# Linear attention and two gated MLPs on one core: one loop over all chunks, the narrow tile fourth in layer one, moved copies

## The reference

```python
q_s = softmax(q, axis=-1); k_s = softmax(k, axis=2)        # exp(. - max) / (sum + 1e-9)
kv = einsum('bhsd,bhse->bhde', k_s, v)
x = einsum('bhsd,bhde->bhse', q_s, kv)  -> [B * S, H * D]
h = x @ w_in;  r = max(h, 0);  x = (s * r * r + b) @ w_out                       # layer one
h = x @ w_in2; sp = log1p(exp(min(h, 20))); out = (h * tanh(sp)) @ w_out2        # layer two
```

## Time and profile before

| | us |
|---|---|
| median of 3 runs | 891.26 (889.41 to 893.04) |
| profiled execution | 890.38 |
| its span, first to last instruction | 888.6 |
| TensorE busy | 865.1 (97%) |
| VectorE busy | 613.5 (69%) |
| ScalarE busy | 378.7 (43%) |
| GpSimd busy | 26.6 (3%) |
| mean granted TensorE clock | 0.988 of full |

### The profile page before, as it was taken

How to read it: one execution, slowest core, us unless ns; L and a number is a source line. 1 busy time by engine, 2 the same in 40 slices (tenths; PEclk the granted TensorE clock), 3 DMA queues, 4 the chain that set the end, 5 groups by cost and what they waited for, 6 DMA issues and landing times.

```text
span 888.6 us, 11126 instructions
## 1 busy us (share of the span) xinstructions
PE 865.1 (97%) x4132; PEld 717.5 (81%) x4132; DVE 613.5 (69%) x1037; ACT 378.7 (43%) x621; POOL 26.6 (3%) x30
## 2 busy tenths in 40 slices
PE   9789999999999999999999899998999999999998
PEld 4578888888888888888997678897888788878886
DVE  8787776665475554222466889688797779778975
ACT  4445433332333323222356555455454445445443
POOL 2300000000000000000000000000000000000000
PEclk9799999999999999999999999999999999999999
DMA  9921111111111100000153000100000000000001
GB/s 227 339 53 40 25 29 28 41 41 41 41 40 40 40 0 1 1 1 0 49 190 143 1 0 1 48 1 1 25 1 0 12 36 0 0 28 19 0 0 48
DMA packets 60645, 36.15 MB, mean 41 GB/s; under 512 B 48320, under 2 KB 50368, under 8 KB 60608
## 3 DMA queue, kind: packets, MB, share of 16 engines
q1 hardware_dynamic: 60608, 35.66, 14.2%
HBM read 30.93 MB, written 4.72 MB: 40 GB/s over the span
## 4 chain that ended last, share of the span: by engine, by line
PE 80%; DVE 11%; ACT 6%; issue 2%; POOL 1%; DMA 0%; DVEq 0%; ACTq 0%
PE H L796 38%; PE Y L810 21%; PE Y L824 17%; PE H L763 2%; PE H L784 2%; ACT t L458 1%; DVE g L702 1%; DVE t L674 1%; ACT t L460 1%; DVE wout_lo L598 1%; DVE t L679 1%; ACT wout_hi L360 1%; DVE t L684 1%; PE H L775 1%; DVE win_lo L598 1%
## 5 line engine op out<-in xcount | busy, mean ns | idle before, releaser
L796 PE MATMUL H<-xs_hi,win_hi 128*128 128x512 f32 (+1 forms) x640 | 240.8, 376 | 7.7 <-DVE g_raw L697 3.3
L796 PE MATMUL H<-xs_hi,win_lo 128*128 128x512 f32 (+1 forms) x640 | 236.8, 370 | 0.0
L796 PE MATMUL H<-xs_lo,win_hi 128*128 128x512 f32 (+1 forms) x640 | 236.7, 370 | 0.0
L824 PE MATMUL Y<-wout_hi,g 128*128 128x512 f32 x576 | 190.1, 393 | 5.4 <-DVE g L702 5.4
L810 PE MATMUL Y<-g,wout_hi 128*128 128x512 f32 (+1 forms) x640 | 183.3, 371 | 0.7 <-DVE g L582 0.7
L796 PEld LDWEIGHTS H<-xs_hi,win_hi 128*128 128x128 f32 x640 | 121.4, 190 | 30.0 <-DVE g_raw L697 4.0
L796 PEld LDWEIGHTS H<-xs_hi,win_lo 128*128 128x128 f32 x640 | 121.3, 190 | 20.8
L796 PEld LDWEIGHTS H<-xs_lo,win_hi 128*128 128x128 f32 x640 | 121.4, 190 | 20.4
L824 PEld LDWEIGHTS Y<-wout_hi,g 128*128 128x128 f32 x576 | 108.7, 189 | 30.9 <-DVE g L702 8.7
L810 PEld LDWEIGHTS Y<-g,wout_hi 128*128 128x128 f32 x640 | 115.2, 189 | 20.1 <-DVE g L582 0.9
L577 DVE SCALAR_TENSOR_TENSOR g_raw<-g_raw,s_col 128x512 f32<-128x512 f32 (+1 forms) x80 | 55.5, 694 | 96.4 <-ACT g_raw L381 96.1
(11 more groups left out here) (73 smaller groups left out, 823.2 us busy)
## 6 DMA issues: line engine op xcount, KB each, us to landing
win_raw<-in_moe_w_in_dram SPq DMA_DIRECT2D x8, 1024.0 KB, 7.0
wout_raw<-in_moe_w_out_dram SPq DMA_DIRECT2D x8, 1024.0 KB, 7.3
g_flat<-in_v_dram SPq DMA_DIRECT2D x32, 144.0 KB, 3.3
out_dram<-xy SPq DMA_DIRECT2D x18, 256.0 KB, 2.1
qbuf<-in_q_dram SPq DMA_DIRECT2D x24, 144.0 KB, 2.8
kbuf<-in_k_dram SPq DMA_DIRECT2D x24, 144.0 KB, 2.9
raw<-in_k_dram SPq DMA_DIRECT2D x4, 288.0 KB, 3.9
raw<-in_q_dram SPq DMA_DIRECT2D x4, 288.0 KB, 6.1
```

The source lines that it names most:

```text
L796: last = nc.tensor.matmul(Hb[f % banks][:, 0:w], a[:, i, cols], m[:, i, 0:w], start=(i == 0 and n == 0), stop=(i == KC - 1 and n == XPASS ...
L824: last = nc.tensor.matmul(Y[i][:, :], g[:, f % LAG_B, a, rows], m[:, f, :], start=(f == 0 and n == 0), stop=(f == FC - 1 and n == XPASS - 1))
```

## The change

- One loop over the chunks c of all ten steps (`SRC` lists the tiles in their order) on ACT, DVE and PE, all unrolled: up(c) is followed by down(c - 3), and by down(c - 4) from the fifth chunk of layer two on, also across tiles. The hardware loops go.
- Layer one's order is 0, 1, 2, 4, 3. The conversions of layer two's weights (`NEXT_HI`, `NEXT_LO`) stay beside its fifth step, which is now the full tile 3.
- `xhi` has two buffers; the lo part is written over x itself (`xlo`). The four splits of the next tile stand beside the chunks of `split_at`.
- Y is copied beside the third (layer two: fourth) chunk of the next step, and the first down of a step waits for it. In layer two VectorE copies bank 1 between `g_lo_b` and `m_of_e` and bank 3 behind `m_of_e`; ScalarE copies its banks ahead of that chunk's logarithm.
- Units start at the chunks in `START`: 0, 4, 7, 10 for batch 1, then 13, 17, 21, 25 and 29, 33, 37, 41. The transposes and kv are three chunks later, x five.
- `take_x` goes from DVE to ACT. `k_max` goes behind `g_lo`, and for the unit at chunk 0 q_max and q_shift too.
- The hi part of w_in 1 goes from ahead of the loop to chunk 0 (`FIRST_HI`); two lo parts come a chunk later.
- `kv_product` makes one product for each head, into its half of the partitions.

```diff
-        FIRST_HI = {2: ('out', 1), 4: ('in', 2), 6: ('out', 2), 8: ('in', 3), 10: ('out', 3)}
-        FIRST_LO = {1: ('in', 1), 3: ('out', 1), 5: ('in', 2), 7: ('out', 2), 9: ('in', 3), 11: ('out', 3)}
+        FIRST_HI = {0: ('in', 1), 2: ('out', 1), 4: ('in', 2), 6: ('out', 2), 8: ('in', 3), 10: ('out', 3)}
+        FIRST_LO = {1: ('in', 1), 3: ('out', 1), 5: ('in', 2), 8: ('out', 2), 9: ('in', 3), 12: ('out', 3)}
...
+        A_ORDER = (0, 1, 2, FULL, 3)
+        SRC = A_ORDER + B_ORDER
...
+                START[FC * (batch - 1) + (0, 4, 7, 10)[p] if batch == 1 else FC * (batch - 1) + (-3, 1, 5, 9)[p]] = (batch, p)
...
+        def split_at(pos, f):
+            steps = (5, 9, 12, 15) if pos == 0 else (5, 8, 11, 14) if pos < TILES else (6, 8, 10, 12)
+            return steps.index(f) if pos + 1 < len(SRC) and f in steps else None
...
             wout_hi_part(0, 0)
-            win_hi_part(0, 1)
             act.wait_ge(sb_in, 32)
...
+            for c in range(FC * TILES):
+                pos, f = c // FC, c % FC
+                if unit_at(c - 5):
+                    take_x(unit_at(c - 5))
+                if pos > 0 and f == LAG_A - 1:
+                    take_y(pos - 1)
+                relu(c, WIDTH[pos])
+                if unit_at(c - 2):
+                    take_qT(unit_at(c - 2))
+                g_hi(c, WIDTH[pos])
+                if unit_at(c):
+                    q_exp(unit_at(c))
+                if unit_at(c - 1):
+                    k_exp(unit_at(c - 1))
+                if pos == 0 and f in FIRST_HI:
+                    kind, i = FIRST_HI[f]
+                    hi_part(kind, 0, i)
...
+                if split_at(pos, f) is not None:
+                    split_hi(pos + 1, split_at(pos, f))
...
+            for c in range(FIRST, END):
+                pos, f = c // FC, c % FC
+                if pos == TILES and f == LAG_A - 1 or pos > TILES and f == LAG_B - 1:
+                    take_y(pos - 1)
+                rough_inverse(c, WIDTH[pos])
+                if c + 1 < END:
+                    exp_h(c + 1, WIDTH[(c + 1) // FC])
+                if c > FIRST:
+                    g_hi_b(c - 1, WIDTH[(c - 1) // FC])
...
-                    last = nc.tensor.matmul(n.bank[0][:, 0:PAIR * VW], n.kj[:, j, :], n.v[:, :, j, :],
-                                            start=(j == 0), stop=(j == J - 1))
+                    for h in range(PAIR):
+                        rows = slice(h * D, (h + 1) * D)
+                        last = nc.tensor.matmul(n.bank[0][rows, 0:VW], n.kj[:, j, rows], n.v[:, h, j, :],
+                                                start=(j == 0), stop=(j == J - 1))
...
+            for c in range(FIRST):
+                if unit_at(c - 5):
+                    x_product(unit_at(c - 5))
+                n = unit_at(c - 3)
+                if n and n.u > NP:
+                    q_transpose(n)
+                if c >= HA:
+                    pe.wait_ge(ha_taken, c - HA + 1)
+                up(c, HA)
+                if n and n.u == NP:
+                    q_transpose(n)
+                elif n:
+                    kv_product(n)
+                if c >= LAG_A:
+                    down_a(c - LAG_A)
+                if n and n.u == NP:
+                    kv_product(n)
```

More of the change, by code:

```diff
@@ L73, in linear_attention_moe_kernel @@
         wout_raw, _ = place("wout_raw", [P, FC, DM], F32, o)
[L75 to L78, removed]
+        xy, o = place("xy", [P, KC, N])
+        xlo, _ = place("xlo", [P, KC, N], F32R, o)
+        xhi = []
+        for half in range(2):
+            here, o = place(f"xhi{half}", [P, KC, TILE], F32R)
+            xhi.append(here)
+            if half == 0:
+                xs_raw, _ = place("xs_raw", [P, KC, TILE], F32, o)
         g, o = place("g", [P, HB, 2, TILE], F32R)
@@ L270, in _ @@
                 load_wout(0, i)
[L271 to L276, removed]
+            for u in range(NP + 1, B * NP):
+                load_unit(Unit(u // NP, u % NP))
             for i in range(NG):
@@ L365, in hi_part @@
                 (win_hi_part if kind == 'in' else wout_hi_part)(layer, i)
[L367 to L374, removed]
@@ L388, in take_y, with take_x @@
[L388 to L392, removed]
+            def take_x(n):
+                for half in range(2):
+                    act.wait_ge(x_done, 2 * n.u + half + 1)
+                    nc.scalar.activation(xy_half[:, n.p, n.b, half, :], n.bank[half][:, 0:HALF],
+                                         ACT.Copy).then_inc(x_taken, 1)
@@ new lines, in split_hi @@
+            def split_hi(pos, i):
+                src, w = SRC[pos], WIDTH[pos]
+                if pos < TILES:
+                    act.wait_ge(x_taken, 2 * (NP * min(pos, B - 1) + i + 1))
+                else:
+                    act.wait_ge(y_taken_act, y_count(A_ORDER.index(src) + 1) // 2)
+                    act.wait_ge(y_taken_dve, y_count(A_ORDER.index(src) + 1) // 2)
+                if pos >= 2:
+                    act.wait_ge(h_ready, FC * (pos - 1))
+                nc.scalar.activation(xhi[pos % 2][:, i, 0:w], xy_tile(i, src, w), ACT.Copy).then_inc(xhi_done, 1)
@@ new lines, in take_y @@
+            def take_y(pos):
+                src, w = SRC[pos], WIDTH[pos]
+                for i in range(0, BANKS[pos], 2):
+                    act.wait_ge(y_ready, y_count(pos) + i + 1)
+                    if pos < TILES:
+                        dst, y = xy_tile(i, src, w), Y[i][:, 0:w]
+                    elif w == TILE:
+                        dst, y = xy_tile(i, src, w), Y[i][:]
+                    else:
+                        dst, y = last_rows(i), Y[i].rearrange("p (a n) -> p a n", n=LAST)
@@ L403, in _ @@
                 if p >= 2:
-                    split_hi(0, 0, x_units=0, parts=[p - 2])
-            split_hi(0, 0, x_units=0, parts=range(NP - 2, NP))
+                    split_hi(0, p - 2)
+            for i in range(NP - 2, NP):
+                split_hi(0, i)
             wout_hi_part(0, 0)
-            win_hi_part(0, 1)
             act.wait_ge(sb_in, 32)
[L410 to L476, removed]
@@ L500, in _ @@
+            g_hi_b(END - 1, WIDTH[-1])
+            take_y(len(SRC) - 1)
         @block.vector
@@ L547, in kv_norm @@
                 bank = n.bank[0]
-                for h in range(PAIR):
-                    rows = slice(h * D, (h + 1) * D)
-                    last = nc.vector.tensor_scalar_add(ksum[rows, n.p, :], bank[rows, (h + 1) * VW - 1:(h + 1) * VW], EPS)
+                last = nc.vector.tensor_scalar_add(ksum[:, n.p, :], bank[:, VW - 1:VW], EPS)
                 last.then_inc(ksum_done, 1)
@@ L660, in _ @@
-            tile_a(0, True)
-            with dve.Fori(1, NEXTRA) as t:
-                tile_a(t, True)
-            for T in (FULL - 1, FULL):
-                tile_a(T, False)
-            def min_e(T, f, w):
-                dve.wait_ge(e_done, FC * T + f + 1)
-                t = t1[:, f % 2, 0:w]
+            for c in range(FC * TILES):
+                pos, f = c // FC, c % FC
+                w = WIDTH[pos]
+                if unit_at(c - 3):
+                    kv_norm(unit_at(c - 3))
+                if pos > 0 and f == LAG_A - 1:
+                    for i in (1, 3):
+                        take_y(pos - 1, i)
+                if unit_at(c) and c > 0:
+                    q_max(unit_at(c))
+                    q_shift(unit_at(c))
+                square(c, w)
+                if unit_at(c - 1):
+                    k_shift(unit_at(c - 1))
+                g_lo(c, w)
+                if unit_at(c):
+                    if c == 0:
+                        q_max(unit_at(c))
+                        q_shift(unit_at(c))
+                    k_max(unit_at(c))
+                    q_sum(unit_at(c))
+                    q_eps(unit_at(c))
+                    q_inv(unit_at(c))
+                    q_scale(unit_at(c))
+                if pos == 0 and f in FIRST_LO:
+                    kind, part = FIRST_LO[f]
+                    lo_part(kind, 0, part)
+                if pos == FULL and f in NEXT_LO:
+                    kind, part = NEXT_LO[f]
+                    lo_part(kind, 1, part)
+                if split_at(pos, f) is not None:
+                    split_lo(pos + 1, split_at(pos, f))
@@ new lines, in g_lo_b @@
+            def g_lo_b(c, w):
+                dve.wait_ge(ghi_done, c + 1)
+                nc.vector.tensor_tensor(g[:, slot(c), 1, 0:w], g_raw[:, slot(c), 1, 0:w],
+                                        g[:, slot(c), 0, 0:w].bitcast(F32), ALU.subtract).then_inc(g_ready, 1)
+            FIRST, END = FC * TILES, FC * len(SRC)
+            for c in range(FIRST, END + 2):
+                pos, f = c // FC, c % FC
+                w0, w1, w2 = [WIDTH[min(c - back, END - 1) // FC] for back in range(3)]
+                if FIRST < c <= END:
+                    rough_ratio(c - 1, w1)
+                if c < END:
+                    min_e(c, w0)
+                if FIRST < c <= END:
```

(33 more changed lines are left out.)

343 lines of the change are left out of this document (128 added, 215 removed).

## The result

The changed kernel takes 880.47 us (median of 4 runs, 879.09 to 881.31) against 890.34 before (four runs, the three of above and one beside them): the ratio of the runs is given as 0.987, interval 0.9852 to 0.9889, and the two medians by themselves stand at 0.989, its upper end. I forecast 885.2, which is 6.1 less than the 891.26 above; the medians show 9.9 less, the ratio 11.6. The profiled execution took 879.09 us, the fastest of the four, with a span of 877.3, so the two traces stand 11.3 apart. (For the kernel before the trace is of a run near the median, so that comparison flatters the change by about a microsecond.)

The account below looks back on a forecast made before the run. TensorE, busy 97% of an 888.6 us span, was taken as the bound; +3.3 - 2.1 - 3.9 - 5.0 - 1.4 (other layer-two boundaries) + 3.0 = -6.1 gave a span of 882.5 and a median of 885.2, range 875 to 895.

Parts of the forecast that it names:

- The kv product: 24 passes over 65 columns replacing 12 over 130: +0.25 us a unit, +3.0 in twelve, between -8 and +14.
- columns streamed: Pricing kv's product by its 1560 columns, the same as before: 1.34 us a unit.
- side by side: Rival: kv's two halves overlap, a gain of 0.67 us a unit, span about 874; chance 0.14.
- the 1.0 that I had named as a sign of being wrong: The forecast is wrong if kv takes under 1.0 us or over 2.5 us a unit.
- The refill that I added: Some restart cost for TensorE around kv's product, counted as +0.25 us a unit.
- Tile 0: Later up(3), +1.4 us, and a wait of 1.6 with 0.3 refill at the tile's end, +1.9: +3.3.
- The narrow tile fourth: Moving layer one's narrow tile ahead of the last full tile removes its whole loss: -2.1 us.
- The first tile of layer two: Interleaved downs cover part of the late weight parts' delay: -3.9 us, with 3.9 of the 7.8 lost staying.
- The narrow tile of layer two: Interleaving tiles removes its starting wait and end splits: -5.0 us, with 0.4 left.
- the microsecond that I had ruled out: No TensorE wait over a microsecond after the two in layer two's first tile.
- The copies of Y: The wait for Y at each tile's head costs no stall; the copies (0.7 us) end under the next up.
- The copies of x, q's order: ScalarE copying x, and q_max and q_shift placed later, cost TensorE nothing.

Follow-up runs that it names:

- Experiment 3: Changed kernel with kv's loops swapped, six products of head 0 and then six of head 1: 886.01 us, ratio 0.9929.
- experiment 5: Changed kernel with the hi part of w_in 1 copied ahead of the loop again: 878.33 us, ratio 0.9841.
- experiment 4: Changed kernel with layer one's narrow tile last again (0, 1, 2, 3, narrow): 884.82 us, ratio 0.9914.
- Experiment 7: Changed kernel with VectorE's layer-two splits one chunk behind ScalarE's: 876.16 us, ratio 0.9819.
- 8: Changed kernel with the four splits beside chunks 0, 1, 2 and 4 of layer two's narrow tile instead of 6, 8, 10 and 12: 883.91 us, ratio 0.9899.
- 9: Changed kernel with ScalarE's layer-two copies of Y behind that chunk's logarithm and exponential instead of ahead: 887.83 us, ratio 0.9961.
- 10: Changed kernel with the copies of x by VectorE again, at the same chunks: 881.16 us, ratio 0.9893.
- experiment 2: Kernel before with only the change to kv's product and what kv_norm reads: 886.67 us, ratio 0.995.
- experiment 11: Changed kernel with w_in 1 copied ahead of the loop, and VectorE's late weight parts and layer-two splits one chunk behind ScalarE's: 871.96 us, ratio 0.9785.

## Why the prediction was wrong, and where it held

**The kv product: the step that failed.** I put +3.0 and it was -3.4: 6.4 us of difference, more than the whole miss in the span (5.2). I took "columns streamed", 1.34, and had side by side as a rival at 0.14. The product took 0.85, under the 1.0 that I had named as a sign of being wrong; the rival's 0.67 was too low too, and with the 0.21 behind it the gain is 0.28 a unit and not the rival's 0.67. Experiment 3 shows that columns streamed was the right price for the wrong order: passes that follow each other in one half take 0.057. In the change they alternate, and take 0.035. Half by half the whole form costs 0.02 + 0.21 a unit over the wide one, 2.8 in twelve, which is my +3.0. The text that I weighed in the one sentence, that tiles can load and multiply in parallel (TensorEngine Tiling (Array Packing), Key Properties, in the Trainium skill), is the one that the runs bear out. What spoke against it, that nothing in the trace overlaps two streams, was no evidence, because nothing in the trace used two halves. The refill that I added exists: the down group behind kv takes 2.94 with the halves in either order and 2.72 or 2.73 with the wide form, 0.21 or 0.22 a unit. By the rule of the same section of the Trainium skill that a change of tiling mode drains TensorE, this would be its price; the runs show the 0.22 and not its cause.

The range had its lower bound for this term at -8 us, so the result lies inside 875 to 895; but the change came out larger than forecast by 1.6 times by the medians and 1.9 by the ratio.

**Tile 0: +3.3, measured +2.8.** relu(1) came behind the w_in copy as worked out: up(3) at 53.33, forecast 53.5; experiment 5 puts the copy's price at about 2. The last split of tile 1 gave 1.16 of wait, forecast 1.6.

**The narrow tile fourth: right**, with no wait in either of layer one's last two tiles, and experiment 4 shows that it is this and not the interleaving alone. One reading beside it was wrong, at no price: I wrote that in the kernel before the next tile's first products run beside the old tile's last. They don't. Four downs stand in a row at a tile's end, with a unit's product among them (132.60 to 144.51). Layer one's boundaries were closed because the next tile's splits fit in under these downs.

**The first tile of layer two: -3.9, measured -4.9.** Two waits, before down(2) and down(5), at 0.74 and 1.60 against 1.0 and 2.3. The chain that I worked out was 0.3 too long by the first and 0.7 by the second.

**The narrow tile of layer two: the second step that failed.** I left 0.4 and 3.2 stayed (0.35, 1.10, 0.87 and the refills); one of them is over the microsecond that I had ruled out. This miss of 2.8 goes the other way, and with the smaller ones it hides part of kv's. I compared sums: VectorE's 44.7 us of the tile before, splits in it, with TensorE's 50. But in the kernel before all four of VectorE's splits came at the tile's end (616.22 to 620.05), where the last g was nearly through, and not one by one in a running chain. As put now each makes VectorE wait for ScalarE's half. I had seen this for the weight parts (2.29 of work cost 5.1) and didn't carry it to the splits. Experiment 7 took it away, and 8 shows that to move them where TensorE's steps are longer is no cure.

**The copies of Y.** I said that the wait for Y costs no stall. One of 0.87 came, in the chain that the splits had delayed (it goes in 7). And I gave the place ahead of the logarithm no value: behind it, 8 us are lost (9).

**The copies of x, q's order.** In the trace the copies make no wait over 0.28 on either engine (10); by time this is known to about 2 us only. q's order was not tried by itself.

## What to carry to other kernels

Two small products in different column halves of the array went at 0.035 us a pass issued in turn, and at 0.057 issued half by half. Put them in turn. When a form isn't in the trace, its price can be on the other side of zero from every row that is.

Where two engines make one thing in two steps (a hi and a lo part), issue the second engine's step a chunk later: an engine that works in program order stands still between them, and here that cost more than the work. Two such shifts gave 3.3 and 4.5 us here, and with the w_in copy moved back 7.6 to 8.5 together, against 9.9 to 11.6 for the whole change. And compare chains and not sums of busy time, wherever an engine that is 80% busy has something inserted.

## What the runs showed of the hardware

Loads and passes of kv's product in the changed kernel: duration in ns, min, median and max, then first and last start.

```profile
L743 PEld LDWEIGHTS H<-g_flat,kbuf x288: 132/138/140, 61.2 to 312.8; 96*64 96x64 f32 x144
L743 PE MATMUL H<-g_flat,kbuf x288: 218/222/272, 61.2 to 312.8; 96*64 96x65 f32 x144
```

A load of 64 columns takes 138 ns against 188 for 128, and none of it shows at a spacing of 0.035 us a pass. The durations are the same, 138 and 222, in experiment 3, where a pass goes every 0.057: the length of a record doesn't tell the rate.

The clock's answer to one and the same wait differs from run to run. The 12 matmuls behind the wait at up(3), with the mean granted clock over them:

| run | wait | the 12 matmuls | granted clock |
|---|---|---|---|
| kernel before | 2.88 | 4.38 | 0.66 |
| experiment 2 | 2.89 | 3.02 | 1.00 |
| experiment 5 | 2.51 | 4.54 | 0.64 |
| experiment 11 | 2.54 | 3.04 | 1.00 |
| changed kernel | 4.19 | 4.61 | 0.63 |
| experiment 3 | 4.20 | 5.49 | 0.51 |

In the kernel before the first of them start 0.43 apart (the level of 1.2 GHz) and the last 0.23 (2.4 GHz). In the changed kernel it is the other way round: the first start 0.24 apart, and from the sixth on, 1.4 us after TensorE began again, it is 0.43. So up to 1.5 us of a single comparison of spans here is the clock. The start of the first up is another 1.4: it lies between 39.71 and 41.09 in the fourteen traces. That is why the ratios above are from several runs.
